# An xLSTM-style attention and mixture kernel: the order of the opening on TensorE, VectorE, ScalarE and GpSimd, and the form of the fourth unit's scores

## The reference

```
m_new  = max(f + m, i);  f_stab = exp(f + m - m_new);  i_stab = exp(i - m_new)
C = f_stab * C + i_stab * outer(v, k);   n = f_stab * n + i_stab * k
x = sigmoid(o) * (C @ q) / max(|n . q|, 1)
p = domain_probs / (sum(domain_probs) + 1e-9)
out = sum over e of p[:, e] * (relu(x @ w1[e]) @ w2[e])
```

## Time and profile before

| what | us |
|---|---|
| median of 3 runs (lowest, highest) | 418.74 (417.88, 418.81) |
| the profiled execution | 418.08 |
| its span | 416.4 |
| TensorE busy | 411.6 |
| VectorE, ScalarE, GpSimd busy | 180.6, 158.5, 152.3 |

### The profile page before, as it was taken

The page is one execution under the profiler, slowest core; times in us unless marked ns, Lnnn a source line. Parts: engine busy times, 40 slices in busy tenths (PEclk is TensorE's granted clock), DMA queues, the critical chain, the costliest instruction groups (busy, mean ns, idle before and its releaser), DMA issues.

```text
span 416.4 us, 7050 instructions
## 1 busy us (share of the span) xinstructions
PE 411.6 (99%) x2710; PEld 398.3 (96%) x2710; DVE 180.6 (43%) x372; ACT 158.5 (38%) x329; POOL 152.3 (37%) x189
## 2 busy tenths in 40 slices
PE   8999999999999999999999999999999999999997
PEld 8899999999999999999999999999999999999996
DVE  5875796646555556446223232323113132311313
ACT  4575477745355653514112431144211333211111
POOL 4865735595174925304011660065100453000000
PEclk9999999999999999999999999999999999999999
DMA  7999939678513845300000231024200000000101
GB/s 269 272 283 394 369 100 354 226 256 290 189 37 131 303 132 193 122 2 0 2 0 2 85 129 67 0 71 139 71 0 2 0 0 2 34 0 2 63 0 65
DMA packets 16899, 48.45 MB, mean 116 GB/s; under 512 B 1921, under 2 KB 8594, under 8 KB 15714
## 3 DMA queue, kind: packets, MB, share of 16 engines
q1 hardware_dynamic: 16290, 46.60, 31.9%
q10 hardware_dynamic: 576, 1.40, 1.0%
HBM read 45.94 MB, written 2.05 MB: 115 GB/s over the span
## 4 chain that ended last, share of the span: by engine, by line
PE 98%; DVE 1%; issue 0%; DVEq 0%
PE hid_ps L1076 42%; PE acc_ps L1095 37%; PE out_ps L1032 5%; PE score_ps L1095 3%; PE acc_ps L1076 2%; PE out_ps L1039 2%; PE score_ps L976 2%; PE add_ps L1011 1%; PE hid_ps L925 1%; PE score_ps L971 1%; PE acc_ps L1032 0%; PE out_ps L1051 0%; PE out_ps L1052 0%; PE out_ps L1053 0%; PE score_ps L989 0%
## 5 line engine op out<-in xcount | busy, mean ns | idle before, releaser
L810 DVE SCALAR_TENSOR_TENSOR h_lo<-hid_ps,h_hi 128x384 fp32r<-128x384 f32 (+2 forms) x120 | 68.0, 567 | 219.7 <-ACT h_hi L587 219.6
L587 ACT ACTIVATE h_hi<-hid_ps 128x384 fp32r<-128x384 f32 (+2 forms) x120 | 59.6, 497 | 231.9 <-PE hid_ps L1076 231.8
L1095 PE MATMUL acc_ps<-w_hi,h_hi 128*128 128x320 f32 x352 | 110.2, 313 | 0.0
L1095 PE MATMUL acc_ps<-w_hi,h_lo 128*128 128x320 f32 x352 | 108.8, 309 | 0.0
L1095 PE MATMUL acc_ps<-w_lo,h_hi 128*128 128x320 f32 x352 | 108.4, 308 | 0.0
L1076 PE MATMUL hid_ps<-xt_hi,w_hi 128*128 128x384 f32 (+2 forms) x360 | 104.1, 343 | 0.1
L1076 PE MATMUL hid_ps<-xt_hi,w_lo 128*128 128x384 f32 (+2 forms) x360 | 103.7, 342 | 0.0
L441 POOL TENSOR_TENSOR w_lo<-w_raw,w_hi 128x384 fp32r<-128x384 f32 x56 | 58.9, 1054 | 114.5 <-ACT w_hi L573 114.5
L1076 PEld LDWEIGHTS hid_ps<-xt_hi,w_lo 128*128 128x128 f32 x360 | 65.4, 189 | 4.3
L1095 PEld LDWEIGHTS acc_ps<-w_hi,h_hi 128*128 128x128 f32 x352 | 66.3, 188 | 1.3
L1095 PEld LDWEIGHTS acc_ps<-w_lo,h_hi 128*128 128x128 f32 x352 | 66.3, 188 | 1.3
(11 more groups left out here) (172 smaller groups left out, 371.9 us busy)
## 6 DMA issues: line engine op xcount, KB each, us to landing
w_raw<-in_w_b SPq DMA_DIRECT2D x27, 704.0 KB, 4.3
raw<-in_qk_s SPq DMA_DIRECT2D x8, 1024.0 KB
g_all<-g_dram SPq DMA_DIRECT2D x10, 512.0 KB, 6.1
kv<-in_kv_n SPq DMA_DIRECT2D x12, 352.0 KB, 5.9
q_pack<-in_q_p SPq DMA_DIRECT2D x10, 192.0 KB, 6.1
out_y<-y_acc SPq DMA_DIRECT2D x12, 160.0 KB, 1.8
carry<-g_dram SPq DMA_DIRECT2D x30, 60.0 KB
y_acc<-in_o_n SPq DMA_DIRECT2D x1, 1280.0 KB, 12.3
```

Of the source, the lines that this page charges most:

```text
L587: nc.scalar.activation(h_hi[:, M % RING, 0:cols], hid_bank(M)[:, 0:cols], ACT.Relu).then_inc(hid_hi, 1)
L810: nc.vector.scalar_tensor_tensor(h_lo[:, M % RING, 0:cols], hid_bank(M)[:, 0:cols], 0.0, h_hi[:, M % RING, 0:cols].bitcast(fp32), ALU.max, ...
L1095: last = nc.tensor.matmul(acc_ps[t][:, 0:DM], x, w, start=(f == 0 and i == 0), stop=(f == NF - 1 and i == 2))
```

## The change

The fourth unit's scores (unit 3) go the way of units 4 to 11: NS is 3, casts stand in slots 3 and 4, subtractions in 4 and 5; its load of 1024 KB (before 256 and 160) is issued by ScalarE in the opening. TensorE's `move_ends` and `move_starts` come ahead of scores, and six products of `keep_clock` stand ahead of `outputs(0)`; the first keys are turned into another bank and copied by ScalarE, and `outputs(1)` waits for the copy of the weights' tokens alone. VectorE takes `unit_maxima` ahead of the first probabilities and `unit_steps` from GpSimd; GpSimd makes the sums ahead of the second weighing of keys. ScalarE splits blocks 2 and 3 ahead of the first `xt_high` and opens the gates of units 2 and 3 between `relu(0)` and `relu(1)`. SyncE asks for weight pair 3 before it waits for the stores. The state keeps 120 rows, for 128 with zeros, and its products take 120, 120 and 80 rows. Three memsets of VectorE and GpSimd fall away.

```diff
@@ -24,7 +24,7 @@
 RAW_PAIRS = 4
-NS = 4
+NS = 3
 KA, Q_ODD = 64 + D, 2 * HALF * L
@@ -38,9 +38,9 @@
 DN_FIRST, DN_END = 0, 20
-CAST = {4: (11, 12), 5: (16, 17), 6: (23, 24), 7: (26, 29), 8: (33, 35), 9: (39, 41), 10: (42, 45), 11: (49, 50)}
-SUB = {4: (13, 14), 5: (18, 19), 6: (25, 27), 7: (29, 30), 8: (35, 37), 9: (41, 43), 10: (45, 46), 11: (51, 53)}
-OPEN_IN = {3: (2,), 13: (4,), 14: (6,), 17: (8,), 18: (10,)}
+CAST = {3: (3, 4), 4: (11, 12), 5: (16, 17), 6: (23, 24), 7: (26, 29), 8: (33, 35), 9: (39, 41), 10: (42, 45), 11: (49, 50)}
+SUB = {3: (4, 5), 4: (13, 14), 5: (18, 19), 6: (25, 27), 7: (29, 30), 8: (35, 37), 9: (41, 43), 10: (45, 46), 11: (51, 53)}
+OPEN_IN = {13: (4,), 14: (6,), 17: (8,), 18: (10,)}
 LATER_PAIRS = {12: 8, 14: 9, 16: 10}
@@ -263,7 +263,7 @@
         def scores_in(k):
-            return 16 * (k // 2 + 1)
+            return 16 * sum(2 if u < NS else 1 for u in range(B + k % 2, k + 1, 2))
@@ -334,16 +334,15 @@
             sp.dma_start(g_dram[1, NU:NU + 1, :], gate_tiles[1]["gg"][0:1, 1, :]).then_inc(gate_tiles[1]["stored"], 16)
-            load_q(3)
+            load_pair(sp, 3)
             sp.wait_ge(gate_tiles[1]["stored"], 3 * 16)
             load_g(2)
+            load_carry(2)
+            load_q(3)
             sp.wait_ge(out_done, 1)
...
             load_kv(sp, 2)
-            load_carry(2)
-            load_pair(sp, 3)
             load_g(3)
-            reload_scores(3)
             sp.wait_ge(out_done, 2)
@@ -387,9 +386,6 @@
             pool.wait_ge(ident_ready, 2)
-            nc.gpsimd.memset(apart[0:64, 1, Q_ODD:Q_ODD + HALF * L], 0.0).then_inc(apart_set[1], 1)
-            nc.gpsimd.memset(apart[64:KA, 1, 0:HALF * L], 0.0).then_inc(apart_set[1], 1)
-            pool.wait_ge(apart_set[1], 2)
             nc.gpsimd.memset(kw[:, :, DM:], 0.0).then_inc(pool_init, 1)
@@ -493,10 +478,9 @@
             causal(1, 1)
-            unit_steps()
             weigh_keys(0)
+            unit_sums()
             weigh_keys(1)
-            unit_sums()
             for w in range(FIRST):
@@ -535,6 +519,13 @@
+            def first_keys():
...
+                gt = gate_tiles[0]
+                act.wait_ge(gt["key_ps"], 1)
+                nc.scalar.activation(key_w[:, 0:U0], hid_ps[0][:, U0:2 * U0], ACT.Copy).then_inc(gt["key_tok"], 1)
...
             def decays(k, half):
@@ -595,13 +586,16 @@
             split_high(1, None)
+            first_keys()
             act.dma_start(y_acc[:, 2:4, :], o_n[:, 2:4, :]).then_inc(o_in[1], 16)
             act.dma_start(dp[:, :, :], dom_p).then_inc(dp_in, 16)
+            load_scores(act, 3)
+            split_high(2, None)
+            split_high(3, None)
             xt_high(0)
             xt_high(1)
-            split_high(2, None)
-            split_high(3, None)
             relu(0)
+            gate_open(2)
             relu(1)
@@ -631,9 +625,8 @@
             nc.vector.memset(ones[:, :], 1.0).then_inc(ones_set, 1)
-            nc.vector.memset(apart[0:64, 0, Q_ODD:Q_ODD + HALF * L], 0.0).then_inc(apart_set[0], 1)
-            nc.vector.memset(apart[64:KA, 0, 0:HALF * L], 0.0).then_inc(apart_set[0], 1)
-            nc.vector.memset(state[96:128, :, 0:H * DA], 0.0).then_inc(rows_set, 1)
+            nc.vector.memset(apart[0:64, 0, Q_ODD:Q_ODD + HALF * L], 0.0).then_inc(apart_set, 1)
+            nc.vector.memset(apart[64:KA, 0, 0:HALF * L], 0.0).then_inc(apart_set, 1)
             nc.vector.memset(g_parts[:, :].bitcast(fp32), 0.0).then_inc(parts_set, 1)
@@ -683,11 +676,11 @@
-            def copy_keys(n, first, rows, bank):
...
-                gt = gate_tiles[n]
+            def later_keys():
...
+                gt = gate_tiles[1]
                 dve.wait_ge(gt["key_ps"], 1)
-                nc.vector.tensor_copy(key_w[:, first:first + rows], bank[:, rows:2 * rows]).then_inc(gt["key_tok"], 1)
+                nc.vector.tensor_copy(key_w[:, U0:NU], out_ps[:, U1:2 * U1]).then_inc(gt["key_tok"], 1)
@@ -729,8 +722,20 @@
+            def unit_steps():
...
+                gt = gate_tiles[1]
+                dve.wait_ge(m_ready, 1)
+                dve.wait_ge(local_ready, 3)
+                nc.vector.tensor_tensor(gt["fm"][:, :], gt["w"][:, :], m_u[:, :], ALU.add).then_inc(unit_step, 1)
+                dve.wait_ge(unit_step, 1)
+                nc.vector.tensor_scalar(gt["g"][:, :], gt["fm"][:, :], 0.0, None, ALU.min).then_inc(unit_step, 1)
+                nc.vector.tensor_scalar(gt["j"][:, :], gt["fm"][:, :], 0.0, -1.0, ALU.max, ALU.mult).then_inc(unit_step, 1)
...
             local_maxima()
             unit_starts()
+            unit_maxima()
@@ -786,8 +791,7 @@
                 else:
-                    dve.wait_ge(rows_set, 1)
-                    target = state[0:KS, k, 0:H * DA]
+                    target = state[:, k, 0:H * DA]
                 nc.vector.tensor_tensor(target, add_bank.get(k, add_ps)[0:KS, 0:H * DA],
@@ -832,12 +836,11 @@
             probs(0, 1)
-            unit_maxima()
             probs(1, 0)
             probs(1, 1)
-            copy_keys(0, 0, U0, acc_ps[2])
+            unit_steps()
+            gate_scan(1)
             gate_x(0)
-            gate_scan(1)
             gate_x(1)
@@ -866,7 +869,7 @@
                 dve.wait_ge(decay_ps, 1)
-                copy_keys(1, U0, U1, out_ps)
+                later_keys()
                 dve.wait_ge(mask_ready, 3)
@@ -1021,7 +1024,7 @@
                 elif k == 1:
-                    pe.wait_ge(gate_tiles[0]["key_tok"], 1)
+                    pe.wait_ge(gate_tiles[0]["w_tok"], 1)
                 elif k == B:
@@ -1106,19 +1109,22 @@
             exponents_first(0, 1)
+            move_ends()
             exponents_first(1, 0)
             exponents_first(1, 1)
-            move_ends()
+            move_starts()
             first_scores(0)
-            move_starts()
             first_scores(1)
+            pe.wait_ge(m_begun, 1)
+            keep_clock(6)
             outputs(0)
...
             pe.wait_ge(g0["w_tok"], 1)
-            turn(g0, "key", acc_ps[2], U0, U0, "key_ps")
+            turn(g0, "key", hid_ps[0], U0, U0, "key_ps")
             outputs(1)
...
             additions(0)
+            pe.wait_ge(g0["key_tok"], 1)
             keep_clock(2)
@@ -1036,8 +1039,8 @@
-                        last = nc.tensor.matmul(bank[:, first * DA:(first + n) * DA], q_pack[:, kept(k), g, :],
-                                                state[:, kept(k), first * DA:(first + n) * DA],
+                        last = nc.tensor.matmul(bank[:, first * DA:(first + n) * DA], q_pack[0:n * D, kept(k), g, :],
+                                                state[0:n * D, kept(k), first * DA:(first + n) * DA],
@@ -1182,7 +1188,7 @@
         "qk_a": apart.reshape(NS, KA, 2 * HALF * L),
-        "qk_s": _np.concatenate([qk, qk[:, 0:24], qk, qk[:, 24:], _np.zeros_like(qk[:, 0:128 - KS])], axis=1).reshape(NT - NS, 128, 2 * H * L),
+        "qk_s": _np.concatenate([qk, qk[:, 0:24], qk, qk[:, 24:], qk[:, 0:128 - KS]], axis=1).reshape(NT - NS, 128, 2 * H * L),
         "q_p": q_p,
...
                                  _np.zeros((NT, L, KV - DM - H * DA), q.dtype)], axis=2),
```

More of the change, by code:

```diff
@@ L155, in build @@
         y_acc, w_raw = landing("y_acc", [L, NT, DM]), landing("w_raw", [128, 2 * RAW_PAIRS, WB])
-        state, fresh = sb("state", [128, B, GROUP * GROUP * DA]), sb("fresh", [KS, GROUP * GROUP * DA])
+        state, fresh = sb("state", [KS, B, GROUP * GROUP * DA]), sb("fresh", [KS, GROUP * GROUP * DA])
         early = y_acc[0:U1, 4:NT, :].rearrange("u n m -> u (n m)")
@@ L231, in build @@
         d_exp, d_masked, p_ready = sem("d_exp"), sem("d_masked"), sem("p_ready")
-        mask_turn, ones_set, apart_set = sem("mask_turn"), sem("ones_set"), [sem(f"apart_set{i}") for i in range(2)]
+        mask_turn, ones_set, apart_set = sem("mask_turn"), sem("ones_set"), sem("apart_set")
         kv_ones, unit_step, first_in = sem("kv_ones"), sem("unit_step"), [sem(f"first_in{i}") for i in range(B)]
@@ L366, in _ @@
                     reload_scores(5)
-                if (k := unit_at(M, -2)) is not None and NS <= k < NT - 2:
+                if (k := unit_at(M, -2)) is not None and NS < k < NT - 2:
                     reload_scores(k + 2)
@@ L461, in carry_state @@
                 pool.wait_ge(pool_init, 3)
-                st = state[0:KS, kept(k), :].rearrange("p (g c) -> p g c", g=GROUP)
+                st = state[:, kept(k), :].rearrange("p (g c) -> p g c", g=GROUP)
                 nc.gpsimd.tensor_tensor(st, st, decay[:, k - B, :].unsqueeze(2).broadcast_to([KS, GROUP, GROUP * DA]),
@@ L465, in carry_state @@
                 pool.wait_ge(state_scaled, k - B + 1)
-                nc.gpsimd.tensor_tensor(state[0:KS, kept(k), :], state[0:KS, kept(k), :], fresh[:, :], ALU.add)\
+                nc.gpsimd.tensor_tensor(state[:, kept(k), :], state[:, kept(k), :], fresh[:, :], ALU.add)\
                     .then_inc(state_ready, 1)
-            def unit_steps():
```

(11 more changed lines are left out.)

4 lines of the change are left out of this document (2 added, 2 removed).

## The result

Before 418.81 us, after 420.31 (medians of 7 and 7 executions, side by side), ratio 1.0063 [1.0038, 1.0089]; a second set of the changed kernel gave 419.42 (12 executions), ratio 1.0034 [1.0016, 1.0052]. The forecast was 417.8 in a range of 416.6 to 419.3: wrong in sign and outside the range. The first ratio is twice what was called no change, the second just above it.

A forecast was written before the change was run, and what follows sets the result against it. TensorE, busy 99%, was taken as the bound, so only its order and waits count: head +0.6, scores -0.92, pair 3 -0.19, pair 4 -0.26, stall +0.15, sum -0.62 us, giving 417.8 us, range 416.6 to 419.3.

The forecast's parts named there:

- Head: Opening up to `up(0)`, at 18.96 us before: `up(0)` starts at 19.55, a cost of +0.6 us.
- The new order: TensorE's opening, `move_ends` and `move_starts` ahead of the first scores: TensorE free at 11.36 instead of 11.46 us.
- the products: Six idle products ahead of `outputs(0)`: 1.4 us long, partly hidden by a wait, `outputs(0)` 1.03 us late.
- Scores of unit 3: Stream behind `up(0)`: a half takes 0.40 us split instead of 0.86 packed, -0.92 us.
- Pair 4: Weight load behind `up(8)`: asked for and landing some 1.5 us earlier, -0.26 us, bounds 0 and -0.26.
- `outputs(3)`: TensorE's wait there for unit 3's last probability, in VectorE's full row: a stall of +0.15 us.
- The step that failed: SyncE's early pair 3 and unit 3's early 1024 KB: scores gone before pair 4, gates' stores given no cost.
- the stream: From `up(0)` on: scores -0.92, pair 3 -0.19, pair 4 -0.26, stall at `outputs(3)` +0.15 us.
- Pair 3: Weight load asked for before the wait on the gates' stores: `up(6)` 0.96 us instead of 1.15, -0.19 us.
- VectorE late with unit 3: Slots 5 to 9: pair 4 no earlier, `outputs(3)` stalls 1.3 to 2.0 us, 419.2 to 419.9; chance 0.15.
- The products cost nothing: Head: something else holds `outputs(0)` or they overlap, it starts near 11.9, sum -1.2, 417.2 us; chance 0.12.
- The clock pays them back: First 18 us: denser order makes every execution like the fast one, up to 0.9 us more, 416.9; chance 0.08.

The follow-up runs named there:

- e2: Changed kernel with weight pair 3 asked for at its old place, behind unit 2's loads: 421.31 us at full clock, ratio 1.0081 to the kernel before.
- e4: Changed kernel with both pair 3 and unit 3's scores asked for by SyncE at their old places: 420.00 us at full clock, ratio 1.0053.
- e10: Changed kernel with unit 3's scores left packed, 416 KB from SyncE, no cast or subtraction for them: 418.31 us at full clock, ratio 1.0003.
- e11: Changed kernel with unit 3's scores asked for late by SyncE and ScalarE's two DMA issues ahead of its keys' copy: 418.60 us at full clock, ratio 1.0019.
- e6: Kernel before with only TensorE's new order, `move_ends` and `move_starts` ahead of the scores: 418.48 us at full clock, ratio 1.0008.
- e1: Changed kernel without its six idle products ahead of `outputs(0)`: 419.73 us at full clock, ratio 1.0038 to the kernel before.
- e13: Changed kernel with TensorE's old order of the opening: 419.25 us, all 12 executions at full clock, ratio 1.0027.
- e17: Changed kernel with unit 3 packed, no idle products, TensorE's old order, `unit_maxima` behind the first probabilities: 417.89 us at full clock, ratio 0.9994.
- e3: Changed kernel with unit 3's scores asked for by SyncE behind `load_g(3)`, not by ScalarE early: 418.52 us at full clock, ratio 1.0020.
- e9: Kernel before with only pair 3 asked for ahead of the wait on the gates' stores: 418.74 us at full clock, ratio 1.0013.
- e7: Kernel before with only the six idle products ahead of `outputs(0)`, in a bank of their own: 419.06 us at full clock, ratio 1.0016.
- e16: Changed kernel with unit 3 packed, no idle products and TensorE's old order: median 421.75 us, all 5 executions at low clock, ratio 1.0079.
- e5: Changed kernel with unit 3's scores asked for late by SyncE and without the six idle products: 418.78 us at full clock, ratio 1.0020.
- e15: Changed kernel with unit 3 packed and without the six idle products: 417.82 us at full clock, ratio 0.9997.
- e8: Kernel before with only unit 3's scores split, 1024 KB loaded by SyncE at the old place: 419.76 us at full clock, ratio 1.0066.
- e18: Changed kernel, unit 3 packed, no products, TensorE's old order, `unit_maxima` behind first probabilities, ScalarE's two DMA issues before its keys' wait: 417.73 us at full clock, ratio 0.9989.

## Why the prediction was wrong

*Head, right in its sum.* Forecast +0.6; the second profile has +0.72, as have e2, e4, e10 and e11. Two of its parts were off and made up for each other. The new order was put at 0.1 earlier and makes `outputs(0)` 0.4 later (e6, e1); the products, put at 1.03 on the path, add 0.8 to that (e1 to the changed kernel). The first profile has +1.07: ScalarE's issue of the domain shares took 1.71 us for the 0.42 assumed, so the splits ended at 19.26 for the 17.9 assumed and `up(0)` waited 0.42 for `xt_high(1)`.

*Scores of unit 3, right.* 0.40 a half, -0.92. *Pair 4*, right by luck: in the first profile it was asked for at 29.13, 2.8 later and not 1.5 earlier, and landed at 35.87 for 36.19. `up(8)` fell to 0.99 since TensorE came to it at 40.67 for 37.87; the wait of ScalarE fell from 4.54 to 1.42 for the same reason and the two casts. The term itself shows where the gates aren't late (e10: `up(6)` 0.96, `up(8)` 0.99). *`outputs(3)`*: no wait, for the 0.15 put there.

*The step that failed* is the one on SyncE's queue, where a term was put at nothing without a reason: pair 3 asked for ahead of the gates' wait, and the scores of unit 3 "issued near 16 us and gone before pair 4 is asked for". It asked what the added megabyte does to pair 4, never what it and pair 3 do to the stores and the load of the gates between them. From the last store's issue to `load_g(2)` it takes 5.0 to 6.5 us in the five profiles with the early megabyte (after 5.9, its second set 5.9, e1 6.5, e2 5.0, e13 5.1), and 2.2 to 4.4 in the thirteen without it whose head ran at full clock (before 2.4, e4 2.6, e17 4.4). With the decays of unit 2 late, GpSimd's `w_lo` is late, and `up(5)` and `up(6)` take 1.3 us more; there the forecast had -0.19. In the means at full clock the stream is +1.06 - 0.72 = +0.34, where -1.22 was forecast: nearly the whole miss of 1.7. Moving that one issue back gives 0.93 (e3), leaving the scores packed 1.14 (e10). So the megabyte's place is shown to cost some 0.9 of it; the rest is the split's own traffic, and pair 3 beside the gates' load (e9, e17).

*Pair 3* was worth its place, but only in this company: without it the changed kernel is 1.9 slower (e2).

*Rivals.* VectorE late with unit 3 did not happen in the changed kernel, since the megabyte came early; it is what the later megabyte brings (0.7 us in e3, 1.2 in e11, 1.8 in e4). So the split has to pay on one side or the other, and its 0.92 was not had by any version here: none with the split is below e10 (418.31) or e15 (417.82). "The products cost nothing" is out by e7. "The clock pays them back" was right that executions differ by how late the opening gets fast: from 4.0 to 6.0 us TensorE starts 6 or 7 records in each half microsecond of the second set and 4 or 5 in the first profile, though the granted clock is given as 1.00 in both. That is the first term of the table, which no edit moves. Behind it the rival had the wrong sign: in the kernel before the clock holds without them (141 of 144). The products guard it only against a wait that the change itself opens (e16 to e13), and they don't guard against the new order's own fall. That the change could lower the clock in one execution of four was no case of the forecast, and it lifts the first median by some 0.65 us (420.31 for 419.66, the median of its four at full clock).

*Open.* No low execution of the changed kernel itself was profiled; that its clock falls where e3's does is inferred from the same order and the same mean. That it is the small products which bring it down, and why in some executions and not in others, no run shows; e1, e5 and e15, with the new order and no products, were low in 9 of 32, but they also have a wait of 0.57 us ahead of `outputs(0)`. And the profiles' +2.0 against the means' +1.06 stays unexplained beyond the spread of single executions.

## What to carry to other kernels

Before a load is put earlier, list what small stores and loads are in flight in that stretch and who waits for their completion: half-idle DMA engines were no proof of room here, since a store of 0.5 KB behind a megabyte was reported 5.9 us after its issue (2.4 before), and its lateness held up three engines. Time saved ahead of a late transfer is lost to it (e1), so mend the transfer first and cut the head after. And count the executions by granted clock beside the median: this reordering cost nothing that was told apart in most of them (e6) and 2 to 4 us in every fourth of the changed kernel.

## What was not expected of the hardware

- The load that waits for a small store went out 2.2 to 4.4 us after the store's issue without, and 5.0 to 6.5 with, a megabyte asked for 0.8 to 2.0 us ahead of it on *another* engine's queue. The Trainium skill ("DMA: Bandwidth & Descriptors", Queues, rings and completion order) has the DMA engines take turns between the queues' rows by the packet; the forecast leaned on that for ScalarE's transfer, and did not turn it round: by the same rule SyncE's stores share each engine with ScalarE's megabyte. The trace agrees with this reading (5.0 us in e2, where SyncE asks for no weights behind the stores); that it is the turns and not the memory behind them no run shows.
- The issue of one small DMA (24 KB) held ScalarE for 0.45 us in e3, 1.33 in e4 and 1.71 in the changed kernel.
- TensorE's granted clock fell to 0.50 with TensorE busy 2.00 of 2.00 us (e3, from 9.8 to 16.6 us), after 1.44 us of idle (e16, from 13.8 to 20.6, and all 5 executions were low), after 1.58 us (e8, from 38.7 to 49.0), and after waits of 0.75 and 0.60 us close together (e18, from 29.6 to 33.0).
- The 24 records of the opening took 4.30 to 5.49 us, and no edit decides which. That is up to 1.2 us of the spread of a kernel's executions (417.0 to 420.1 us for the kernel before).
